# Attention scores contracted over all 128 rows, with the query parts doubled by on-chip transfers

## The reference

```python
# 1. linear attention for 8 batches, 8 heads, 576 rows, head size 64
kv  = einsum('bhsd,bhse->bhde', k, v)
out = einsum('bhsd,bhde->bhse', q, kv)
x   = out / sqrt(mean(out*out, -1) + 1e-6) * g_norm          # then (B, S, 512)
# 2. mixture of 4 attention experts, the best 2 of each row
logits = x @ w_gate;  w = softmax of the top 2
for e in range(4):
    q = x @ wq[e];  k = x @ wk[e];  v = x @ wv[e]             # 64 columns each
    scores = q @ k.T / sqrt(64), causal mask, softmax         # 576 x 576
    out += (w of e where chosen) * (a @ v @ wo[e])
# 3. gated block
h = gelu_tanh(x @ w_in);  u, v = halves of h
v_n = layer norm of v, times g_ln
v_s = w_sg @ v_n + b_sg
y = x + (u * v_s) @ w_out
```

## Time and profile before

| | |
|---|---|
| runs | 911.61, 914.76, 914.87 us (median 914.76) |
| profiled execution | 911.67 us |
| its span | 909.9 us, 17540 instructions |
| mean granted TensorE clock | 0.998 |
| TensorE matmul busy | 878.0 us, 96% of the span |
| VectorE / ScalarE / GpSimd busy | 459.7 / 410.6 / 181.5 us |

### The profile page before, as it was taken

How to read it: one execution, slowest core, us unless ns; L and a number is a source line. 1 busy time by engine, 2 the same in 40 slices (tenths; PEclk the granted TensorE clock), 3 DMA queues, 4 the chain that set the end, 5 groups by cost and what they waited for, 6 DMA issues and landing times.

```text
span 909.9 us, 17540 instructions
## 1 busy us (share of the span) xinstructions
PE 878.0 (96%) x7009; PEld 764.5 (84%) x7009; DVE 459.7 (51%) x1221; ACT 410.6 (45%) x978; POOL 181.5 (20%) x213
## 2 busy tenths in 40 slices
PE   6898999999999999999999999999999999999898
PEld 4686898979988798977989789897998879897796
DVE  1567723475345743377334772347534674337730
ACT  1457523474335633465244652347433563336521
POOL 0402233002420034101330023300342003410130
PEclk9999999999999999999999999999999999999999
DMA  9902313003030032100330030300303000000001
GB/s 278 233 1 67 108 36 93 12 2 105 6 99 1 1 106 58 49 1 8 99 82 24 1 82 25 93 12 2 106 7 99 2 2 1 23 31 1 1 1 53
DMA packets 77648, 45.76 MB, mean 50 GB/s; under 512 B 54592, under 2 KB 70976, under 8 KB 77568
## 3 DMA queue, kind: packets, MB, share of 16 engines
q1 hardware_dynamic: 77568, 44.63, 18.6%
HBM read 35.19 MB, written 9.44 MB: 49 GB/s over the span
## 4 chain that ended last, share of the span: by engine, by line
PE 79%; DVE 9%; ACT 8%; SPq 2%; issue 1%; DMA 1%; POOL 0%; POOLq 0%; ACTq 0%; DVEq 0%
PE w L887 38%; PE t L887 19%; ACT probs L581 5%; PE t L941 4%; PE t L1033 4%; PE w L926 3%; DVE neg_max L698 3%; PE t L957 3%; DVE probs L719 2%; PE t L1022 2%; PE w L1085 2%; PE t L1041 2%; PE t L973 2%; ACT work L596 1%; DVE yT L829 1%
## 5 line engine op out<-in xcount | busy, mean ns | idle before, releaser
L887 PE MATMUL w<-wout_s,big 128*128 128x512 f32 x480 | 119.2, 397 | 1.6 <-DVE big L747 1.6
L887 PE MATMUL t<-big,wqk_s 128*128 128x288 f32 x768 | 111.4, 301 | 0.9 <-DVE big L815 0.6
L887 PEld LDWEIGHTS w<-wout_s,big 128*128 128x128 f32 x480 | 89.3, 188 | 22.0 <-DVE big L747 2.1
L887 PE MATMUL w<-wsgT_s,big 128*128 128x288 f32 x768 | 107.7, 296 | 0.0
L887 PEld LDWEIGHTS t<-big,wqk_s 128*128 128x128 f32 x768 | 104.4, 190 | 1.8 <-issue 1.5
L887 PEld LDWEIGHTS w<-wsgT_s,big 128*128 128x128 f32 x768 | 104.3, 189 | 0.0
L581 ACT ACTIVATE probs<-w,neg_max 128x64 f32<-128x64 f32 (+4 forms) x160 | 83.0, 526 | 46.6 <-DVE neg_max L698 43.6
L497 POOL TENSOR_TENSOR var_eps<-bn,eps_t 128x1 f32<-128x1 f32 x40 | 13.3, 333 | 415.4 <-DVE bn L735 414.7
L596 ACT ACTIVATE work<-t 128x384 f32<-128x384 f32 (+3 forms) x160 | 63.1, 450 | 44.5 <-PE t L941 42.7
L941 PE MATMUL t<-ident,probs 128*128 128x128 f32 x480 | 72.5, 282 | 8.0 <-DVE probs L719 6.9
L620 ACT ACTIVATE work<-w 128x512 f32<-128x512 f32 x40 | 23.9, 597 | 118.9 <-PE w L887 118.9
(11 more groups left out here) (106 smaller groups left out, 1414.0 us busy)
## 6 DMA issues: line engine op xcount, KB each, us to landing
kin<-in_k_dram SPq DMA_DIRECT2D x8, 1024.0 KB, 6.3
vin<-in_v_dram SPq DMA_DIRECT2D x8, 1024.0 KB, 8.8
qin<-in_q_dram SPq DMA_DIRECT2D x32, 256.0 KB, 4.8
out_dram<-work SPq DMA_DIRECT2D x32, 256.0 KB, 2.1
staged_win<-in_moe_w_in_dram SPq DMA_DIRECT2D x4, 512.0 KB, 5.3
staged<-in_moe_w_sg_dram SPq DMA_DIRECT2D x4, 288.0 KB, 3.8
kin<-in_k_dram SPq DMA_DIRECT2D x8, 128.0 KB, 2.8
vin<-in_v_dram SPq DMA_DIRECT2D x8, 128.0 KB, 7.0
```

Of the source, the lines that this page charges most:

```text
L887: last = nc.tensor.matmul(o, stationary(hs, c), mv(hm, c), start=c == of[0] and p == 0, stop=c == of[-1] and p == len(PASSES) - 1)
```

## The change

The scores are contracted over all 128 partitions. For head a of a pair, a new tensor `k_stack` holds the HI part of its keys on the head's own 64 partitions and their LO part on the other 64. The query's HI part and LO part must then stand on both halves. ScalarE and VectorE write them on the head's own half of `big2[:, :, 2m + a]`, and a transfer from SBUF to SBUF copies them to the other half. A block of scores is then two passes for each head, with query HI and query LO: four matmuls of 128 rows. The term LO*LO, which was left out, is now included.

ScalarE and VectorE do each qk unit in two instructions of 64 partitions. `k_stack` shares its memory with the front of `staged`; the staged `w_sg` moves to `qT_uT`, and its load waits for the last `o` unit of the first linear attention instead of for kv. SyncE issues eight more transfers in a batch.

```diff
+        with nc.sbuf_tensor("k_stack", [P, 2, EP, S], F32R) as k_stack:
+            pass
         staged = sb("staged", [P, FC * D + SP], F32)
...
+        q_doubled = {(m, h): sem(f"q_doubled_{m}_{h}") for m in range(EP) for h in range(2)}
...
-        wsg_st = [staged[:, SP * t:SP * (t + 1)] for t in range(4)] + [vin[:, 0:SP]]
+        wsg_st = [qT_uT[:, t, :] for t in range(4)] + [vin[:, 0:SP]]
...
+            def double_q(b):
+                for h in range(2):
+                    for m in range(EP):
+                        cols = slice(PAD + HALF * h, PAD + HALF * (h + 1))
+                        u.wait_drained(sp, b, ("qk", (m, h)))
+                        for a in range(2):
+                            there, here = slice(HD * (1 - a), HD * (2 - a)), slice(HD * a, HD * (a + 1))
+                            x = big2[:, :, 2 * m + a, cols]
+                            sp.dma_start(as_f32(x[there, :, :]), as_f32(x[here, :, :])).then_inc(q_doubled[m, h], 16)
...
-            u.wait_full(sp, -1, ("kv", 0))
+            u.wait_full(sp, -1, ("o", NT - 1))
             for t in range(4):
                 sp.dma_start(wsg_st[t][:, PAD:SP], w_sg[P * t:P * (t + 1), :]).then_inc(w_loaded["wsg"], 16)
...
             load_q(1)
+            double_q(0)
...
             for i in range(B - 2):
+                if i > 0:
+                    double_q(i)
...
+            double_q(B - 2)
             store(B - 2, range(NT))
+            double_q(B - 1)
             store(B - 1, range(NT))
...
-                        x = staged[:, 0:4 * SP].rearrange("p (t n) -> p t n", t=4)
-                        nc.gpsimd.tensor_copy(x[:, :, 0:PAD], x[:, :, PAD:2 * PAD])
+                        nc.gpsimd.tensor_copy(qT_uT[:, :, 0:PAD], qT_uT[:, :, PAD:2 * PAD])
...  (ScalarE, qk)
-                        nc.scalar.activation(big2[:, HI, m, PAD + HALF * h:PAD + HALF * (h + 1)], src(U)[:, 0:HALF],
-                                             ACT.Copy, scale=HD ** -0.5 if m < EP else 1.0).then_inc(qk_hi, 1)
+                        x = src(U)
+                        for a in range(2):
+                            rows = slice(HD * a, HD * (a + 1))
+                            if m < EP:
+                                y = big2[rows, HI, 2 * m + a, PAD + HALF * h:PAD + HALF * (h + 1)]
+                            else:
+                                y = k_stack[rows, a, m - EP, HALF * h:HALF * (h + 1)]
+                            nc.scalar.activation(y, x[rows, 0:HALF], ACT.Copy,
+                                                 scale=HD ** -0.5 if m < EP else 1.0).then_inc(qk_hi, 1)
...  (VectorE, qk: twice the instruction of L815, each on 64 partitions; for keys it writes k_stack[there, a, ...])
...  (TensorE, scores)
-                    u.wait_drained(pe, part, ("qk", (e, int(last_col > PAD + HALF))))
+                    for h in range(2):
+                        if P * t - PAD < HALF * (h + 1) and last_col > PAD + HALF * h:
+                            pe.wait_ge(q_doubled[e, h], count(part, 32, 32))
...
-                        for p, (hs, hm) in enumerate(PASSES):
+                        for hs in (HI, LO):
                             for a in range(2):
-                                rows = slice(HD * a, HD * (a + 1))
...
                                 last = nc.tensor.matmul(
-                                    ps[slot][:, o:o + w], big2[rows, hs, e, P * t:P * (t + 1)],
-                                    big2[rows, hm, EP + e, PAD + k0:PAD + k0 + w], start=p == 0 and not end,
-                                    stop=p == len(PASSES) - 1, skip_group_check=True)
+                                    ps[slot][:, o:o + w], big2[:, hs, 2 * e + a, P * t:P * (t + 1)],
+                                    k_stack[:, a, e, k0:k0 + w], start=hs == HI and not end,
+                                    stop=hs == LO, skip_group_check=True)
```

More of the change, by code:

```diff
@@ L813, in body @@
                         cols = slice(PAD + HALF * h, PAD + HALF * (h + 1))
[L814 to L818, removed]
+                        for a in range(2):
+                            here, there = slice(HD * a, HD * (a + 1)), slice(HD * (1 - a), HD * (2 - a))
+                            dve.wait_ge(qk_hi, count(part, 16, 2 * QK_NTH[j] + a + 1))
+                            if m < EP:
+                                hi, lo = big2[here, HI, 2 * m + a, cols], big2[here, LO, 2 * m + a, cols]
+                            else:
+                                keys = slice(HALF * h, HALF * (h + 1))
+                                hi, lo = k_stack[here, a, m - EP, keys], k_stack[there, a, m - EP, keys]
+                            last = nc.vector.scalar_tensor_tensor(
+                                out=lo, in0=ps[u.slot(part, U)][here, 0:HALF], scalar=HD ** -0.5 if m < EP else 1.0,
+                                in1=as_f32(hi), op0=ALU.mult, op1=ALU.subtract)
+                        give(last, U)
                     elif kind == "s":
@@ L926, in scores @@
                                 last = nc.tensor.matmul(
-                                    ps[slot][:, o:o + w], big2[rows, hs, e, P * t:P * (t + 1)],
-                                    big2[rows, hm, EP + e, PAD + k0:PAD + k0 + w], start=p == 0 and not end,
-                                    stop=p == len(PASSES) - 1, skip_group_check=True)
-                                if end and p == len(PASSES) - 1 and (a == 1 or len(score_slots(n)) == 2):
+                                    ps[slot][:, o:o + w], big2[:, hs, 2 * e + a, P * t:P * (t + 1)],
+                                    k_stack[:, a, e, k0:k0 + w], start=hs == HI and not end,
+                                    stop=hs == LO, skip_group_check=True)
+                                if end and hs == LO and (a == 1 or len(score_slots(n)) == 2):
                                     finish(last, V)
```

## The result

The change makes the kernel slower: 920.90 us (median of 5, 919.29 to 921.60) against 911.96 (5 runs, 911.07 to 914.87). The ratio is 1.0087 with a 95% interval of 1.0066 to 1.0108. The forecast was 914.0 and no measurable change. The profiled execution took 921.6 us, its span is 919.8, 9.9 us more than before.

The account below looks back on a forecast made before the run. TensorE was taken to bound the kernel (busy 96%, 79% of the chain). 911.67 - 2.1 (later batches) + 1.5 + 1.3 - 0.2 (start, batch 0) = 912.2, 915.3 taken from the median; stated 914.0, range 908 to 922.

Parts of the forecast that it names:

- What bounds the kernel: Batch attention: chain on TensorE through s4, then ScalarE and VectorE until s8; shorter s5 to s7 only lengthen t4's wait.
- The matmuls' price: Score blocks: 128-row matmuls cost columns plus 0.017 us, 0.11 for 64 or 192 columns; about 0.3 us won a batch.
- Rival 1: Scores: narrow matmuls load weights almost free and a 128-to-64-row passage cost goes; about 910 us, chance 0.19.
- s8: Score unit late in a batch: two blocks of 0.59 us each become 0.55 each, 0.09 us won.
- ScalarE and VectorE in a later batch: Doubled qk instructions add by estimate 0.3 and 0.4 us a unit, covered; costed at nothing, else up to 0.3 a batch.
- The transfers in a later batch: Doubled query for s0: 0.4 us to issue, 2.1 to landing, 0.8 us of cover; s5's have 0.6 to spare.
- Rival 2: Doubled query lands late at s0 in every batch; seven batches lose 0.9 us each, 920.3 us, chance 0.21.
- TensorE waits for the transfers in every batch: A sign, stated in advance, that the forecast is wrong; only one wait, about 2 us before batch 0's s0, was expected.
- The start: Start and batch 0: 1.5 us from late transfers plus 1.3 from doubled instructions, less 0.2 from the scores.
- q in the queue: Batch 0's doubled query lands about 52.3 behind earlier loads, 2.2 us late for s0; net 1.5 us (0.5 to 2.5).
- Rival 3: Stall at s0 in batch 0 lowers TensorE's clock: 1.7 us more, or 917 with a 3 us stall; chance 0.08.
- The doubled instructions in batch 0: Chain passes qk instructions three times on ScalarE and once on VectorE: 1.3 us more (0.4 to 1.7).

Follow-up runs that it names:

- e3: Kernel before, with the six score matmuls of 64 rows replaced by four of 128 rows, layout unchanged (scores wrong): 904.01 us, ratio 0.9904.
- e10: Kernel before, with each mask matmul of 128 rows done as two of 64 rows per head, nothing else of the change: 907.90 us, ratio 0.9960.
- e5: Kernel of e1 with one ScalarE and one VectorE instruction of 128 partitions per qk unit, transfers and wide matmuls kept (scores wrong): 906.29 us, ratio 0.9927.
- e4: Changed kernel with scores again in three passes of 64 rows, transfers and doubled instructions kept: 924.38 us, ratio 1.0129.
- e9: Kernel of e1 with qk(1,1) and qk(2,1) exchanged, both second-half query units right behind s1: 915.78 us, ratio 1.0042.
- e1: Changed kernel with load_q(1) issued behind batch 0's eight transfers instead of ahead of them: 916.41 us, ratio 1.0046.
- e6: Changed kernel without the 64 transfers and the waits for them, both heads reading one query tile (scores wrong): 915.54 us, ratio 1.0040.
- e2: Kernel before, with only the w_sg load's wait moved from unit kv to the last unit o, so later start loads come late: 912.61 us, ratio 0.9992.

## Why the prediction was wrong

**The number.** The sum had 0.5 us more than before, measured were 8.9 (9.9 between the profiled executions). The stated 914.0 held 1.8 us more, for the median of the three runs; in the comparison the kernel before took 911.96, so they belonged to no part of the change. That 920.90 lies inside 908 to 922 is luck: the upper end stood there for transfers late in every batch, and the loss came in the start.

**What bounds the kernel** held for the kernel before: in e3 0.68 of the 0.93 us are won by s4, and in e10, where s5 gets shorter, the wait at t4 grows from 0.54 to 0.68 us. It didn't hold for the kernel after, whose chain runs over ScalarE and VectorE from s2 to s4; its wait at t4 is gone, and t3 has one of 0.55.

**The matmuls' price** was mis-sized, in my disfavour. For wide blocks the form of 128 rows was priced at 0.82 us for 448 columns and took 0.91; for 288 columns at 0.55 and took 0.62 to 0.64 (0.71 for a second block behind its masks). I had added 0.017 us a matmul from the qk units, and found more: 0.91 / 4 is 0.227, of which the columns are 0.187. For 64 columns 0.44 was right, for 192 it was 0.50 (292.38 to 292.88). What the sum left out is the time ahead of them: I priced the six matmuls and never asked about the 0.21 us between the mask's start and theirs, which stand in the same timeline. The change makes it 0.09 to 0.10. Rival 1 named that passage, with a chance of 0.19, and 0.6 us a batch for it and for cheaper narrow matmuls; the passage was worth more, and the narrow matmuls nothing. With that the form wins 0.93 us a batch (e3) where the sum had 0.28. s8, forecast to win 0.09 by its matmuls, takes 1.42 us before and after.

**ScalarE and VectorE in a later batch** is the step that failed first: "I cost it at nothing; without that cover it is up to 0.3 us a batch". With the matmuls of 128 rows in both, the doubled instructions cost 0.97 us (107.93 against e5's 106.96). I counted back-to-back instructions as overlapping; two of them take 0.92 us on VectorE, from 293.34 to 294.27, no less than twice one (0.46). And I looked only at t1. Four in a row stand ahead of the row maximum of s2, two ahead of s3's and s4's, and each delay is handed on to the next, as the chain shows. The two errors cancel, and the batch came out only 0.33 us from the forecast: luck. The four kernels give the whole picture, in us for a batch:

| | 64 rows | 128 rows |
|---|---|---|
| one instruction for a qk unit | 107.88 (before) | 106.96 (e5), 106.95 (e3) |
| two | 108.20 (e4) | 107.93 (after) |

The gain of the wide form is 0.93 where TensorE sets the chain, and 0.27 where VectorE does.

**The transfers in a later batch** held, barely: 2.4 us to landing against the 2.1 taken and 0.61 to issue against 0.4, so that in batch 2 the second (issued from 279.55) lands some 0.1 us before s0 starts at 282.05, and not 0.8. The landing in SBUF is no earlier than that of the stores in DRAM (2.1). Rival 2 (late by 0.9 us in each of seven batches) happened in one of them, by 0.56 us. s5, which was to have 0.6 us to spare, waits in all seven; "TensorE waits for the transfers in every batch" was a sign of being wrong, and it came, but e5 puts its cost in an ordinary batch at nothing.

**The start** is the step that made the result. The sum had 1.5 + 1.3 - 0.2 = 2.6 us, and it was 9.0. Its parts can be measured, each from the last x transposes of the start (40.98 in the earlier trace rows, 41.15 after) to the load in batch 0:

| kernel | from, to | us |
|---|---|---|
| before | 40.98, 106.28 | 65.3 |
| e5: transfers, wide, single, q behind | 43.52, 107.72 | 64.2 |
| e9: as e1, queries first, clock 1.00 after 44 us | 40.37, 107.76 | 67.4 |
| e1: doubled instructions, q behind | 40.33, 109.56 | 69.2 |
| after: q ahead | 41.15, 115.32 | 74.2 |

- q in the queue: 74.2 - 69.2 = 5.0 us, forecast 1.5. I let the doubled query land at 52.3, at most 53; it was 55.3. I had added up the bytes ahead of it, and left out that SyncE's own issue is held up behind the q loads: 2.45 us for the first transfer, and the second isn't even issued before. Then came the low clock. Rival 3 was right in its mechanism with a chance of 0.08: 4.66 us of waiting, then 0.50, and v0 to v3 took 8.30 - 6.02 = 2.3 us more. It should have been tied to the first: whoever forecasts a wait of 2.2 us with an end of 3 has forecast a part of it. The 5.0 are a lower bound, since e1's own start holds 1.0 us of low clock (below); against e6, which has no transfers, s1 comes 5.6 us later (64.47 - 41.15 against 58.33 - 40.63).
- The doubled instructions in batch 0: 67.4 - 64.2 = 3.2 us, forecast 1.3. 1.4 of it lie before v0 starts (11.29 us against 9.93) and 1.8 behind. The forecast counted the ones on the chain of before; the chain moved to others. (e9 also exchanges two qk units, so this figure holds two things.)
- The matmuls of 128 rows: 65.3 - 64.2 = 1.1 us less, forecast 0.2.
- The clock: e1 takes 1.8 us more than e9. 1.0 of it lies before v0, where the clock in e1 is low for about twice as long (6.8 against 3.4 us, my estimate from the windows). The two kernels are the same up to there, and e2, without any doubled instruction, shows the same (0.62 and 0.53 from 40 and 44 us), so this is no cost of the change. The other 0.8 comes at 68.78, where twelve matmuls take 2.52 us instead of 1.85 behind waits of 0.76 and 0.95 us. e9 has the same two waits and no lower clock. What decides it stays open.

The windows of e1 and then of e9, columns as in the earlier trace rows:

```profile
40.00:44.00 4.00, 3.67 (x16) 3.67 (x17) 1.68 (x3) 0.69 (x1) 0.76 (x3) 0.50 1.02 316
44.00:48.00 4.00, 3.93 (x24) 3.73 (x23) 2.51 (x5) 2.75 (x6) 0.00 (x0) 0.78 0.55 145
```
```profile
40.00:44.00 4.00, 3.63 (x17) 3.62 (x18) 1.73 (x3) 0.69 (x1) 0.80 (x3) 0.57 0.96 309
44.00:48.00 4.00, 3.22 (x25) 3.01 (x23) 3.21 (x6) 3.71 (x7) 0.00 (x0) 1.00 0.64 172
```

## What to carry to other kernels

Before TensorE's instructions are made fewer, look at what stands between them: here the passage between 128 and 64 rows was worth more than the passes, and half of it can be had without the change's transfers and doubled instructions (e10). Count the passages on both sides: one that is taken away behind a group can come back ahead of it. An edit that halves the partitions of an instruction on ScalarE or VectorE and doubles their number cost the full double here (0.41 and 0.46 us each, as with 128 partitions), and was free only where no instruction of the chain stood behind it. A transfer that something waits for belongs ahead of large loads in a shared queue (e1), and its time to issue has to be counted beside the bytes in front.

## What the hardware did that I had not expected

- A mask of two bf16 matmuls of 128 rows and 128 columns followed by matmuls of 64 rows: 0.21 to 0.22 us from start to start; followed by 128 rows, 0.09 to 0.10; as four of 64 rows ahead of 64 rows, 0.09 to 0.10. With 64 columns it is 0.16 before, 0.07 after.
- Issuing a transfer of 64 partitions from SBUF to SBUF takes SyncE 0.61 us, more than a store (median 0.36), and 2.45 us behind the q loads.
- The time of the kernel before goes with its mean granted clock: of the 21 runs beside e9 and e10, ten at 0.998 took 910.7 to 911.4 us, eight at 0.996 912.0 to 914.1, three at 0.994 914.9 to 915.7.
